# Keys and queries kept without their rows of zeros, each load in two transfers

## What is computed

```python
# attention, state S of 48 x 48 for each of the 32 (batch, head) pairs
k_n = k / (norm(k) + 1e-6)
for t in range(768):
    y[t] = q[t] @ S
    S = S + beta[t] * outer(k_n[t], v[t] - k_n[t] @ S)
x = y as 3072 x 384
h = relu(x @ w_in);  x1 = (h * h) @ w_out            # 384 -> 2048 -> 384
out = (silu(x1 @ w_gate) * (x1 @ w_val)) @ w_out2    # 384 -> 1536 -> 384
```

## Time and profile before

| | us |
|---|---|
| three runs | 1034.65, 1034.86, 1036.29 |
| median | 1034.86 |
| the profiled execution's own time | 1036.29 |
| its span, first to last instruction | 1034.5 |
| outside the span (1036.29 - 1034.5) | 1.8 |
| TensorE busy with matrix products | 972.1 (94%) |
| mean granted TensorE clock, of full speed | 0.997 |
| DMA, mean over the span | 83 GB/s |

### The profile page before, as it was taken

The page is one execution under the profiler, slowest core; times in us unless marked ns, Lnnn a source line. Parts: engine busy times, 40 slices in busy tenths (PEclk is TensorE's granted clock), DMA queues, the critical chain, the costliest instruction groups (busy, mean ns, idle before and its releaser), DMA issues.

```text
span 1034.5 us, 24141 instructions
## 1 busy us (share of the span) xinstructions
PE 972.1 (94%) x10692; PEld 807.2 (78%) x10692; DVE 415.5 (40%) x693; ACT 306.7 (30%) x599; POOL 216.3 (21%) x342
## 2 busy tenths in 40 slices
PE   2179899999999999999999999999999999999998
PEld 2168789778777877877888888888888888888887
DVE  3976644634643554453266422321321312312222
ACT  2225333332433332332255421211211211212211
POOL 1188283482284087000000000000000000000000
PEclk9999899999999999999999999999999999999999
DMA  6656657456344523612153100100100100100000
GB/s 217 196 158 179 170 149 182 111 129 162 98 118 121 148 72 99 139 68 54 32 204 132 50 12 1 61 1 1 62 1 1 61 1 1 62 1 1 31 1 30
DMA packets 115544, 85.67 MB, mean 83 GB/s; under 512 B 89776, under 2 KB 94512, under 8 KB 115440
## 3 DMA queue, kind: packets, MB, share of 16 engines
q1 hardware_dynamic: 109776, 76.79, 26.3%
q10 hardware_dynamic: 5664, 7.34, 2.3%
HBM read 63.14 MB, written 20.97 MB: 81 GB/s over the span
## 4 chain that ended last, share of the span: by engine, by line
PE 91%; DVE 4%; DMA 2%; issue 1%; ACT 1%; ACTq 0%; SPq 0%; DVEq 0%
PE bank L1059 91%; DVE first_tinv L463 1%; DVE first_prod L460 1%; DVE h_lo L1018 1%; DMA tri_scratch<-gram 0%; DMA first_tri<-tri_scratch 0%; DMA k_dim<-in_kt 0%; ACT h_hi L782 0%; DVE w_lo L997 0%; DMA inv_scratch<-first_tinv 0%; DMA inv<-inv_scratch 0%; ACT gram L804 0%; DVE norm L924 0%; ACT k_sq L815 0%; PE bank L1233 0%
## 5 line engine op out<-in xcount | busy, mean ns | idle before, releaser
L1059 PE MATMUL bank<-x_hi,w_hi 128*128 128x512 f32 (+1 forms) x768 | 293.2, 382 | 1.2 <-DVE x_lo L993 1.2
L1059 PE MATMUL bank<-x_lo,w_hi 128*128 128x512 f32 (+1 forms) x768 | 289.2, 377 | 0.0
L1059 PE MATMUL bank<-x_hi,w_lo 128*128 128x512 f32 (+1 forms) x768 | 289.1, 376 | 0.0
L1059 PE MATMUL bank<-h_hi,w_hi 128*128 128x512 f32 (+1 forms) x552 | 211.4, 383 | 4.1 <-DVE h_lo L1018 3.1
L1059 PE MATMUL bank<-h_hi,w_lo 128*128 128x512 f32 (+1 forms) x552 | 205.1, 372 | 4.2 <-issue 4.2
L1059 PE MATMUL bank<-h_lo,w_hi 128*128 128x512 f32 (+1 forms) x552 | 205.0, 371 | 0.0
L1038 DVE TENSOR_TENSOR stage<-bank,stage 128x512 f32<-128x512 f32 x72 | 49.8, 692 | 318.5 <-ACT stage L889 318.5
L1059 PEld LDWEIGHTS bank<-x_hi,w_hi 128*128 128x128 f32 x768 | 144.9, 189 | 28.9 <-DVE x_lo L993 1.5
L1059 PEld LDWEIGHTS bank<-x_hi,w_lo 128*128 128x128 f32 x768 | 144.9, 189 | 26.4
L1059 PEld LDWEIGHTS bank<-x_lo,w_hi 128*128 128x128 f32 x768 | 145.0, 189 | 25.4
L1012 DVE TENSOR_TENSOR stage<-stage,bank 128x512 f32<-128x512 f32 (+1 forms) x112 | 68.5, 612 | 195.2 <-ACT stage L861 194.9
(11 more groups left out here) (98 smaller groups left out, 559.3 us busy)
## 6 DMA issues: line engine op xcount, KB each, us to landing
w_raw<-in_w SPq DMA_DIRECT2D x12, 576.0 KB, 3.7
k_dim<-in_kt SPq DMA_DIRECT2D x12, 512.0 KB, 4.6
q_dim<-in_qt SPq DMA_DIRECT2D x12, 512.0 KB, 4.0
k_prep<-in_kt SPq DMA_DIRECT2D x10, 512.0 KB, 4.3
x1s<-in_w ACTq DMA_DIRECT2D x12, 384.0 KB, 5.1
k_sq<-in_ky SPq DMA_DIRECT2D x12, 384.0 KB, 3.6
v_tok<-in_vy SPq DMA_DIRECT2D x12, 384.0 KB, 3.1
x_in<-x_scratch SPq DMA_DIRECT2D x6, 768.0 KB, 5.0
```

Of the source, the lines that this page charges most:

```text
L1059: return pe.matmul(dst, lhsT, rhs, start=start, stop=stop, **kw)
```

## The change

Host side: the arrays `kt` and `qt` go from (12, 128, 1024) with zeros to (12, 2, 48, 1024) without. Device side: one transfer of 128 rows of 4 KB becomes two of 48 rows of 4 KB, into the same places of the same tiles. The tiles keep 128 partitions, and the rows between are never written. Each load raises its semaphore by 32 where it raised it by 16, so the waits of G, QK and KS count in steps of 32. Nothing else moves.

```diff
-    NCH, P, _ = kt.shape
+    NCH, P = kt.shape[0], 128
...
+        def load_rows(eng, tile, rows, loaded):
+
+            for r in range(2):
+                eng.dma_start(tile[dims(r), :, :].rearrange("p h t -> p (h t)"), rows[r]).then_inc(loaded, 16)
...
-                sp.dma_start(k_prep[:, :, :].rearrange("p h t -> p (h t)"), kt[n]).then_inc(kp_loaded, 16)
+                load_rows(sp, k_prep, kt[n], kp_loaded)
...
-                sp.dma_start(k_dim[:, :, :].rearrange("p h t -> p (h t)"), kt[n]).then_inc(kd_loaded, 16)
+                load_rows(sp, k_dim, kt[n], kd_loaded)
...
-                sp.dma_start(q_dim[:, :, :].rearrange("p h t -> p (h t)"), qt[n]).then_inc(q_loaded, 16)
+                load_rows(sp, q_dim, qt[n], q_loaded)
...
-            act.dma_start(k_prep[:, :, :].rearrange("p h t -> p (h t)"), kt[1]).then_inc(kp_loaded, 16)
+            load_rows(act, k_prep, kt[1], kp_loaded)
...
-                        pe.wait_ge(kd_loaded, 16)
+                        pe.wait_ge(kd_loaded, 32)
                     else:
-                        pe.wait_ge(kp_loaded, 16 * n)
+                        pe.wait_ge(kp_loaded, 32 * n)
...
-                    pe.wait_ge(kd_loaded, 16 * (n + 1))
-                    pe.wait_ge(q_loaded, 16 * (n + 1))
+                    pe.wait_ge(kd_loaded, 32 * (n + 1))
+                    pe.wait_ge(q_loaded, 32 * (n + 1))
...
     def by_dim(x):
-        out = np.zeros((n, 2, 64, 2, 4, 2, t), x.dtype)
-        out[:, :, :d] = parts(x).transpose(4, 3, 6, 0, 2, 1, 5)
-        return out.reshape(n, 128, 16 * t)
+        return parts(x).transpose(4, 3, 6, 0, 2, 1, 5).reshape(n, 2, d, 16 * t)
```

## The result

The change makes the kernel slower: 1039.32 us median (8 runs) against 1036.03 us (8 runs of before on the same chip), ratio 1.0032 with a 95% interval of 1.0021 to 1.0043, or +3.3 us. The forecast was 1034.0 within 1030.5 to 1037.0. It started from the median of three runs, 1034.86; over eight, before takes 1036.03. Moved up by that 1.2 us, the range would end at 1038.2 and the time would still lie above it. The profiled execution took 1038.78 us, its span 1037.0.

What follows compares the result with a forecast made beforehand. TensorE's work, 91% of the span, was taken as the bound, leaving DMA only the start and one hole. Terms -0.6 + 0 - 0.3 = -0.9 us took the median 1034.86 to 1034.0 us, range 1030.5 to 1037.0.

Steps and rivals of the forecast that it cites:

- The first load: At the start, k_dim beside k_prep: fewer bytes make G(0) earlier, -0.6 us, bounds -0.7 and +1.4.
- Rival B: Pairs into 48 partitions slower than one into 128, at start, hole and N1(1): +2.5 us, 1037.4, chance 0.09.
- What follows the first load: G(0) through the inverse exchange to unit 0: each begins when its predecessor ends, so the 0.6 us carry on.
- From 97 to 113 us: Extra issue ahead of the flipped loads that N1(1) awaits: 0.45 us slack covers it, 0, bounds 0 and +0.45.
- The hole: TensorE's gap at 118.4 to 122.6 us, a code fetch behind bulk loads: shrinks to about 3.9 us, -0.3.
- Rival A: The hole mostly closes, fetch ahead of bulk loads and no clock fall: say 1030.5 us, chance 0.17.
- The later loads: Loads after the first stage, hidden behind TensorE's 99.08 of 100 us: cost nothing and save nothing.
- Rival C: Nothing reaches the end; first load bound by its fixed part, hole by packet-to-use time: 1034.9 us, chance 0.22.

Runs made afterwards that it cites:

- startonly: Kernel before with only the first k_dim and first k_prep loads in two transfers of 48 rows: 1037.92 us, ratio 1.0018.
- halves64: Kernel before with each load as two transfers of 64 rows, zeros included: 1041.60 us, ratio 1.0058.
- shapes: Kernel before with loads of various shapes added on SyncE from 594 us, DMA engines nearly idle: one profiled execution, 1037.15 us.
- swap: Changed kernel with the two transfers of ScalarE's first k_prep load in the other order: 1038.25 us, ratio 1.0019.
- lasttwo: Kernel before with only k_prep 4 and k_dim 1 in two transfers of 48 rows: 1037.41 us, ratio 1.0017.
- latepairs: Kernel before with only the loads issued after 60 us in two transfers of 48 rows: 1036.41 us, ratio 1.0007.
- late: Kernel before with four bulk loads issued only when N2(1) is done: 1034.84 us, ratio 0.9988.
- crossedlate31: Kernel before, first two loads in pairs crossed over the queues, four loads after N2(1), N2(1) moved to slot 31: 1032.45 us, ratio 0.9972.
- aftercrossed: Changed kernel with its first two pairs crossed over the two queues: 1038.35 us, ratio 1.0023.
- earlypairs: Kernel before with only the loads issued from 16 to 42 us in two transfers of 48 rows: 1037.15 us, ratio 1.0009.
- startwhole: Changed kernel with the first k_dim and first k_prep loads whole again, 128 rows each: 1038.73 us, ratio 1.0022.
- rows112: Kernel before with each load one transfer of 112 rows, only the last 16 zero rows left out: 1038.76 us, ratio 1.0020.
- crossedlate: Kernel before, first two loads in pairs crossed over the queues, four loads issued after N2(1): 1034.80 us, ratio 0.9991.

## Why the prediction was wrong

**The first load: the step that failed.** It was sized as -0.6 us: 256 KB less at 380 GB/s. It measured +2.0 us at G(0), and +1.9 us in time by itself (startonly). The rate was taken from transfers of 128 partitions, and the row with the right partitions, the stores of `y_dim`, was set aside for its 256-byte rows. It was the right row: the bound from it, +1.4 us for two pairs at once, was still too low by 0.6. The forecast followed the byte count because no row showed a load of this shape; halves64 and shapes show that bytes were not the limit. The Trainium skill's rule, which the prediction quoted against the change (SBUF — State Buffer, "Can I just issue two DMAs to hit both halves?"), was right in its direction, and the estimate made from its rates, 2.0 against 1.6 us for a pair alone, agrees in its difference with the 4.0 against 3.6 us that shapes and the earlier trace rows give. That transfers to the two halves serialize is too strong for two queues: on opposite halves they moved 187 GB/s (swap) and on the same half 148, if also far from the 273 of whole transfers.

**Rival B** had the mechanism, its place and nearly its price (+2.5 us, 1037.4), with a chance of 0.09. Its signs came at the start: G(0) past 6.5, a landing over 4 us, and `k_dim`'s pair landing 2.0 us later than the single load did, where over 0.6 was to decide. Alone a pair was only 0.4 us longer: the loss comes from two pairs side by side, in the same order of halves (swap). That its sum came near is in part luck. Its first term was 0.6 us too low, the hole went down by 0.4 us and not up by 0.7, N1(1) didn't wait, and the exchange's 0.8 us was not in it.

**What follows the first load.** The 2.0 us were carried on, as the step says of its 0.6. That the exchange takes the same time was wrong: +0.7 to 0.8 us, from the last two pairs of SyncE's queue (lasttwo). No step considered it.

**From 97 to 113 us.** Taken as 0, bounds 0 and +0.45. In the changed kernel no wait of N1(1) shows; in latepairs, where the start is on time, it is 0.4 us. The bound was right. The +0.5 us from U(0) to N1(1) in the changed kernel remains unexplained; 0.4 of it arise between 97.7 and 107.8 us, where the chain has one gap of 0.22 us marked "issue", at 101.35.

**The hole.** Its cause is shown by late and crossedlate31. The forecast of -0.3 us agrees with 4.6 to 4.2 us in sum, which is luck: as one gap of 3.9 us it was wrong, since the fetch of the block before was caught too. Sum and split differ from kernel to kernel, 2.21 + 1.95 here, 2.79 + 2.03 in aftercrossed, 0.66 + 5.60 in latepairs. Rival A did not come.

**The later loads** are hidden in the profile: 99.19 of 100 us busy. The step was right to charge nothing there. Rival C's ground, TensorE's 94%, holds, but its claims that the first load is bound by a fixed part and that nothing reaches the end don't.

The parts, 1.9 (startonly), 0.9 (earlypairs) and 0.7 (latepairs), add up to 3.5 us for a measured 3.3, but each is known to about 1 us only and the last two aren't told from nothing, so the sum proves little. But startwhole and aftercrossed, which should show only the last two, are at +2.3 and +2.4 us, and rows112 at +2.1 with 0.3 us of the start's loss. What is shown is the start's cost; the exchange's 0.7 us is seen in the profiles and argued to come from the last loads of the queue. Something of 0.5 to 1 us in kernels whose loads are not whole stays open.

## What to carry to other kernels

Count the rate of a DMA by the fullest group of partitions that each single transfer reaches, not by its bytes: padding inside a full 128-partition transfer can be free, and taking it out by splitting the transfer can cost. Where pairs of half transfers can't be avoided, put the two queues on opposite halves at each moment, and both halves of the tile that is needed first in front; that makes the first tile early, not the pairs fast. Where TensorE goes through hundreds of small products within a few microseconds, look for gaps marked "issue" 256 instructions apart, keep bulk loads out of the stretch and put long products between the bursts.

## What the runs showed of the hardware

From the issue of the inverse's store to that of the load that waits for it took 2.03 to 2.06 us where the transfer ahead of the store on the same queue had 48, 64 or 112 rows, and 2.38 us where it had 128, in all 17 kernels. Nothing here explains it.

TensorE's granted clock differs between executions of nearly the same program. Here is the stretch from 53 to 65 us in startonly, at 1.2 GHz, where before and after had 1.00:

```profile
53.00:65.00 12.00, 7.81 (x276) 7.26 (x280) 8.36 (x12) 1.09 (x3) 10.70 (x17) 0.50 0.60 154
```

Behind the gaps it differs too. From 118 to 136 us the mean was 0.81 before, 0.91 in late and 0.72 in crossedlate, which has nearly the gaps of late (1.27 + 2.04 us for 1.35 + 2.04). At half speed while it is low, and where TensorE is busy all the while, these are 3.4, 1.6 and 5.0 us of lost time (less by what falls into a gap), a spread larger than what late changed in the gaps (1.2 us).

The runs of the kernel before spread over 1033.7 to 1040.0 us, so one profile can't price 1 us in the end-to-end time; the start of G(0) can be read to 0.1 us.
